# Experts two to four: the first product of two token tiles by seven block products in place of eight

## The reference

```python
def _moe_ref(x, domain_probs, w1, w2):        # N, D, E, F = 1152, 512, 4, 1024
    p = domain_probs / (domain_probs.sum(-1, keepdims=True) + 1e-09)
    out = np.zeros((N, D), dtype=np.float32)
    for e in range(E):
        h = np.maximum(x @ w1[e], 0.0)
        out += p[:, e:e + 1] * (h @ w2[e])
    return out.astype(np.float32)

def _moe2_ref(x, w_in, w_out):                # d_ff = 2048
    h = x @ w_in
    g = h * np.cos(h)
    return (g @ w_out).astype(np.float32)
```

## Time and profile before

| | us |
|---|---|
| median of three runs | 654.84 |
| the profiled execution | 654.78 |
| its span, first to last instruction | 653.0 |
| TensorE busy with matmuls | 642.1 |
| weight loads of TensorE | 576.5 |
| VectorE busy | 259.6 |
| ScalarE busy | 235.7 |
| GpSimd busy | 163.6 |
| granted TensorE clock | 1.000 of full |

### The profile page before, as it was taken

One profiled execution on the slowest core, in us unless ns is written; L12 is line 12 of the kernel. 1 busy time (PEld: TensorE's weight loads), 2 busy tenths in 40 slices (PEclk: granted clock), 3 DMA queues, 4 the chain that ended last, 5 costly groups with the idle time before them and its releaser, 6 DMA issues.

```text
span 653.0 us, 10127 instructions
## 1 busy us (share of the span) xinstructions
PE 642.1 (98%) x3728; PEld 576.5 (88%) x3728; DVE 259.6 (40%) x638; ACT 235.7 (36%) x514; POOL 163.6 (25%) x222
## 2 busy tenths in 40 slices
PE   7899999999999999999999999999999999999998
PEld 5787889999999999999999999998999999999996
DVE  6755321212121212121212122316766576767664
ACT  6676311232111133111133111137554567644552
POOL 6683200154000154000055000068300049500000
PEclk9999999999999999999999999999999999999999
DMA  9865100033000044000034000023200003001011
GB/s 288 258 196 150 68 0 1 6 126 127 1 1 0 1 129 128 0 0 0 0 100 153 6 0 1 1 66 106 86 1 1 1 33 97 2 0 48 0 49 48
DMA packets 21892, 37.21 MB, mean 57 GB/s; under 512 B 2784, under 2 KB 14048, under 8 KB 21856
## 3 DMA queue, kind: packets, MB, share of 16 engines
q1 hardware_dynamic: 20688, 36.71, 17.7%
q10 hardware_dynamic: 1168, 0.02, 0.1%
HBM read 34.36 MB, written 2.36 MB: 56 GB/s over the span
## 4 chain that ended last, share of the span: by engine, by line
PE 96%; DVE 2%; issue 1%; ACT 1%; DMA 1%; POOL 0%; SPq 0%; DVEq 0%
PE bank L865 46%; PE bank L892 45%; PE bank L857 2%; PE bank L821 1%; PE bank L841 1%; DVE arena L613 1%; PE bank L911 1%; DMA arena<-in_k 1%; ACT arena L440 0%; DVE arena L690 0%; DVE arena L628 0%; ACT x_hi L453 0%; POOL arena L387 0%; DVE arena L633 0%; SPq L248 0%
## 5 line engine op out<-in xcount | busy, mean ns | idle before, releaser
L361 POOL TENSOR_TENSOR w_lo<-w_raw,w_hi 128x128 fp32r<-128x128 f32 (+2 forms) x180 | 138.1, 798 | 370.5 <-ACT w_hi L471 368.4
L865 PE MATMUL bank<-x_hi,w_hi 128*128 128x384 f32 (+1 forms) x576 | 196.9, 342 | 0.0
L865 PE MATMUL bank<-x_hi,w_lo 128*128 128x384 f32 (+1 forms) x576 | 194.7, 338 | 0.0
L865 PE MATMUL bank<-x_lo,w_hi 128*128 128x384 f32 (+1 forms) x576 | 193.5, 336 | 0.0
L892 PE MATMUL bank<-w_hi,hp_hi 128*128 128x512 f32 x432 | 170.9, 396 | 0.1
L892 PE MATMUL bank<-w_hi,hp_lo 128*128 128x512 f32 x432 | 170.3, 394 | 0.0
L892 PE MATMUL bank<-w_lo,hp_hi 128*128 128x512 f32 x432 | 168.1, 389 | 0.0
L647 DVE SCALAR_TENSOR_TENSOR hp_lo<-bank,hp_hi 128x384 fp32r<-128x384 f32 x96 | 53.3, 557 | 264.4 <-ACT hp_hi L476 264.4
L476 ACT ACTIVATE hp_hi<-bank 128x384 fp32r<-128x384 f32 x96 | 46.9, 491 | 278.1 <-PE bank L865 275.8
L865 PEld LDWEIGHTS bank<-x_hi,w_hi 128*128 128x128 f32 x576 | 108.3, 188 | 7.1 <-issue 1.0
L865 PEld LDWEIGHTS bank<-x_lo,w_hi 128*128 128x128 f32 x576 | 108.3, 188 | 4.9
(11 more groups left out here) (55 smaller groups left out, 346.2 us busy)
## 6 DMA issues: line engine op xcount, KB each, us to landing
w_raw<-in_weights SPq DMA_DIRECT2D x43, 512.0 KB, 3.6
arena<-in_q SPq DMA_DIRECT2D x12, 192.0 KB, 4.8
result<-arena SPq DMA_DIRECT2D x9, 256.0 KB, 2.1
w_raw<-in_weights SPq DMA_DIRECT2D x8, 256.0 KB, 6.3
arena<-in_k SPq DMA_DIRECT2D x8, 224.0 KB, 5.9
arena<-in_v SPq DMA_DIRECT2D x4, 384.0 KB, 5.1
arena<-in_v SPq DMA_DIRECT2D x4, 320.0 KB, 8.1
arena<-in_k SPq DMA_DIRECT2D x4, 192.0 KB, 3.6
```

Source lines behind the costliest of these rows:

```text
L361: last = nc.gpsimd.tensor_tensor(w_lo[:, f, at:at + part], raw[:, at - begin:at - begin + part], w_hi[:, f, at:at + part], ALU.subtract)
L865: last = nc.tensor.matmul(ps[:, 0:TOK], w[:, f, chunk(c)], x[:, c, token_cols(t)], start=c == 0 and i == 0, stop=c == DC - 1 and i == 2)
```

## The change

For experts 2 to 4 (e = 1 to 3) the first product of tiles 0 and 1 is taken for two chunks of features at once, by Strassen's method in Winograd's form. A is the two chunks' weights (rows: chunk 2g, chunk 2g + 1; columns: the first and second half of the 512 inner elements), B is x (rows: the halves; columns: tile 0, tile 1). Seven products of [256 inner] x [128 features] x [384 tokens], each 2 pieces x 3 matmuls, give the four cells (chunk, tile). The eight products of the kernel before were these 2 x 2 cells of 12 matmuls. The third tile is still done alone, and the first expert and the dense block keep their form.

- **Sums of x (T)**: 10 sums of 128x768 and 4 low parts of that size on POOL, 4 roundings on ACT (`t_high`), once, in the first expert's second and third turns. The fourth overwrites `x_hi` and `x_lo` of tile 1's first half.
- **Sums of weights (S)**: per pair of chunks ("group") 4 sums of 128x256 in place in `w_raw` (`sum_weights`), 2 roundings of 128x512 on ACT (`high_sums`), 4 low parts of 128x256 on POOL (`low_sums`). A slot is loaded again only after its sums are split (`ex_lo_done`). POOL's `low_weights` for the experts is cut from 1024 columns to 256.
- **Combining**: the products alternate between banks 0 and 1. ACT copies the first to `h_raw` (`keep_first`), DVE adds the other six in seven instructions (`add`, L924). ReLU and rounding read `h_raw` (`pair_high`, L630), and so does `pair_low` (L908), now with both operands in SBUF.
- **Second product**: tile 0 sums up in banks 2, 3 and 7, tile 1 in banks 4, 5 and 6, nine matmuls per cell as before. Tile 0's and tile 1's results are taken in the third tile's turn, the third tile's in the next expert's first group, or, after the last expert, in the dense block's start.
- **Third tile**: `pe_alone` runs up in banks 0 and 1 and down two chunks behind. Its last two downs stand in the next expert's first group, or between the dense block's first ups.

The core of the diff:

```diff
-            with pe.Fori(1, E - 1) as e:
-                with pe.Fori(0, NTOK - 1) as t:
-                    pe_turn(e, t, e * NTOK + t)
-                pe_turn(e, NTOK - 1, e * NTOK + NTOK - 1)
-            pe_turn(E - 1, 0, MIX - NTOK)
-            for t in range(1, NTOK):
-                pe_turn(E - 1, t, MIX - NTOK + t, inputs=True)
+            with pe.Fori(1, E - 1) as e:
+                pe_pairs(e)
+                pe_alone(e)
+            pe_pairs(E - 1)
+            pe_alone(E - 1, inputs=True)
+
+            pe.wait_ge(x2_lo_done, OC)
+            for f in range(LAG):
+                pe.wait_ge(w_lo_done, E * FC + f + 1)
+                if f < 2:
+                    pe.wait_ge(hp_lo_done, MIX * FC - 1 + f)
+                up_cells(h_ps[f], f, 0, range(DC)).then_inc(up_done, 1)
+                if f < 2:
+                    down(FC - 2 + f, MIX * FC - 2 + f, None)
             pe_turn(E, 0, MIX, inputs=True)
...
+            def pair_product(g, j, left, right):
+                for c in range(2):
+                    (a_hi, a_lo), (b_hi, b_lo) = left(c), right(c)
+                    for i, (a, b) in enumerate(((a_hi, b_hi), (a_hi, b_lo), (a_lo, b_hi))):
+                        last = nc.tensor.matmul(bank[(g * PRODUCTS + j) % 2][:, 0:TOK], a, b,
+                                                start=c == 0 and i == 0, stop=c == 1 and i == 2)
+                last.then_inc(pair_up, 1)
...
+                    pair_product(g, 0, a11, b11)
+                    pe.wait_ge(ex_lo_done, ex_count(e, g, 0))
...
+                    pair_product(g, 1, s2, t2)
+                    if g == 0:
+                        down(FC - 2, alone(e - 1) * FC + FC - 2, None)
+                    else:
+                        pair_outputs(e, g - 1, 2)
+                    pe.wait_ge(ex_lo_done, ex_count(e, g, 1))
+                    pe.wait_ge(first_kept, kept_count(e, g))
+                    pair_product(g, 2, s1, t1)
+                    pe.wait_ge(pair_taken, product_count(e, g, 0))
+                    pair_product(g, 3, a12, b21)
+                    if g == 0:
+                        down(FC - 1, alone(e - 1) * FC + FC - 1, None)
+                    else:
+                        pair_outputs(e, g - 1, 3)
+                    pe.wait_ge(pair_taken, product_count(e, g, 1))
+                    pair_product(g, 4, s4, b22)
+                    pe.wait_ge(pair_taken, product_count(e, g, 2))
+                    pair_product(g, 5, s3, t3)
+                    pair_outputs(e, g, 0)
+                    pe.wait_ge(w_lo_done, e * FC + (2 * g + 2))
+                    pe.wait_ge(pair_taken, product_count(e, g, 3))
+                    pair_product(g, 6, a22, t4)
+                    pair_outputs(e, g, 1)
...
+            def high_sums(e, g):
+                act.wait_ge(s_summed, e * (GROUPS * 4) + (4 * g + 4))
+                for half in range(2):
+                    nc.scalar.activation(ex_hi[:, g, half * DM:(half + 1) * DM], w_raw[:, (2 * g + half) % STAGE, 0:DM],
+                                         ACT.Copy).then_inc(ex_hi_done, 1)
...
+                for g in range(GROUPS):
+                    keep_first(e, g)
+                    pair_high(e, g, 0)
+                    if g + 1 < GROUPS:
+                        high_sums(e, g + 1)
+                    pair_high(e, g, 1)
+                    pair_high(e, g, 2)
+                    if g < 2:
+                        high_weights(4 + 2 * g, e, alone(e - 1))
+                    pair_high(e, g, 3)
+                    if g < 2:
+                        high_weights(5 + 2 * g, e, alone(e - 1))
...
+            for i in range(LAG):
+                if i < LAG - 1:
+                    times_cosine(i, MIX * FC + i, i > 0)
+                else:
+                    times_cosine(i, MIX * FC + i, True, take_last_of_experts)
```

More of the change, by code:

```diff
@@ L134, in build @@
[L134 to L148, removed]
+        acc = sb("acc", [P, NTOK, DC * TOK])
@@ new lines, in act_alone @@
+            def act_alone(e, sums):
+                for f in range(FC):
+                    alone_high(e, f)
+                    if not sums:
+                        if f >= LAG:
+                            high_weights(f - LAG, e + 1, alone(e))
+                    elif f in (3, 4, 5):
+                        high_weights(f - 3, e + 1, alone(e))
+                    elif f == 6:
+                        high_sums(e + 1, 0)
+                    elif f == 7:
+                        high_weights(3, e + 1, alone(e))
+                    if not sums and f >= 2:
+                        next_input_high(f - 2)
@@ L510, in act_turn @@
                         continue
[L512 to L518 removed]
+                    refill = (f - 1, e + 1, turn) if refills and f > 0 else None
+                    cosine(g, s, True, refill)
                     if inputs and f in TURNS:
@@ L521, in act_turn @@
                 if refills:
[L522 removed]
+                    high_weights(FC - 1, e + 1, turn)
             exponentials(0, 0)
@@ L678, in take_outputs, with dve_alone @@
+            def dve_alone(e, inputs=False):
+                for f in range(FC):
+                    hidden_low(f, alone(e) * FC + f, bank[f % 2])
+                    if f == 0:
+                        take_pair_tile(e, SECOND_TILE)
+                    elif f == 1:
+                        take_pair_tile(e, FIRST_TILE)
+                    if inputs and f >= 2:
+                        next_input_low(f - 2)
             def take_outputs(e, turn, t, last=False):
@@ new lines, in pe_alone @@
+            def pe_alone(e, inputs=False):
+                for f in range(FC):
+                    if f < 2:
+                        pe.wait_ge(pair_taken, product_count(e, GROUPS - 1, 5 + f))
+                    else:
+                        pe.wait_ge(hp_lo_done, alone(e) * FC + (f - 1))
+                    up_cells(bank[f % 2], f, NTOK - 1, range(DC)).then_inc(up_done, 1)
+                    if f < 2:
+                        pair_outputs(e, GROUPS - 1, 2 + f)
+                    else:
+                        down(f - 2, alone(e) * FC + f - 2, tile_taken(e, SECOND_TILE))
+                    if inputs and f >= 2:
+                        turn_input(f - 2)
```

460 lines of the change are left out of this document (349 added, 111 removed).

## The result

| | before | after |
|---|---|---|
| median | 655.16 us (5 runs, 654.76 to 656.16) | 650.68 us (5 runs, 649.98 to 652.42) |
| ratio | 1 | 0.9932, 95% interval 0.9915 to 0.995 |
| profiled execution | 654.78 us, span 653.0 | 650.12 us, span 648.2 |

The changed kernel is faster by 0.7%, or 4.5 us. The prediction was 644.2 us with a range of 642.0 to 647.0, so the sign was right and 5.9 us of the profiled execution's time were not foreseen.

A forecast was written before the change was run, and what follows sets the result against it. TensorE, busy 98% of the span, was taken to bound the kernel, so each removed matmul gives back its whole spacing: 654.78 - 12.64 (matmuls removed) + 2.05 (wait at the dense block's start) = 644.2 us, range 642.0 to 647.0.

The forecast's parts named there:

- What is removed: Groups of experts 2 to 4: 72 first-product matmuls of 384 columns go, at 0.1756 us each, a gain of 12.64 us.
- What stays: Second products: still 9 matmuls for each chunk and tile, a step taken at 2.06 us, with no cost added.
- Rival E: Products of six matmuls are spaced wider: 0.03 us more for each of 504, 15 us, 659 in all; chance 0.02.
- Inside a group: Groups of 15.6 us: bank and cell hand-overs have 1.5 to 2.3 us of slack, so they cost nothing.
- Rival B: Round trips bind in the groups: each of 12 waits some 0.3 us, 647.8 us in all; chance 0.09.
- GpSimd: Some 105 us more GpSimd work; tightest at an expert's first use of the weight sums, slack 1.5 us, cost nothing.
- Rival C: GpSimd is late by up to 3 us at each expert's first product needing its sums: 645 to 647 us; chance 0.08.
- rival D: GpSimd runs lock VectorE's `pair_low` out, 4 us in each of 9 groups: 36 us, 680 in all; chance 0.03.
- The start of the dense block: A down waits 2.27 us for VectorE's take (2.37 with a slower first matmul); net cost 2.05 us.
- U: The end of the third dense chunk's up on TensorE; the down waiting for VectorE's take was to begin 4.38 us later.
- The sum: Whole kernel: 654.78 - 12.64 + 2.05 = 644.2 us, against the profiled execution's own time.

## Why the prediction was wrong, point by point

- **What is removed: right.** 72 matmuls fewer, the first product's spacing unchanged, a run of six in 1.06 us as the earlier trace rows had it.
- **What stays: the step that failed.** "Second products stay at 9 for each chunk and tile" was true of their number, and the sum silently kept their 2.06 us. They took 2.10, as `hp` had moved by 32 bytes against `w` and `x`. The sum lacked a term, for which no row of before gave a price: 4.9 us by the medians with and without the move (650.68 - 645.8). The profiled executions differ by 4.25 us, or by 4.6 from VectorE's `x_lo` row near 84 us to the end; ahead of it the second one ran its first 20 us at a granted clock of 0.91. Rival E spoke of wider spacing, but of the products of six, and at 0.02.
- **Inside a group: right in kind.** TensorE waits nowhere in them. Against 15.61 us a group took 15.78, and 15.66 with `hp` in its old place, so 12 x 0.05 = 0.6 us are left over. Rival B would have shown waits and did not come.
- **GpSimd: right.** 269.0 - 163.6 = 105.4 us more, against 105. The first low sums began at 140.32, 0.7 us a piece, so the first two were ready at 141.7; TensorE took the first of their products at 143.41. Slack 1.7 us, against 1.5. Rival C did not come.
- **`pair_low` and rival D: right for the instruction looked at.** The row below gives 0.59 us on average, and the longest took 1.01, within 0.55 to 1.3. But the block was looked for only in `pair_low`. The copy of shares stood at 85.16 in the trace of before, and the text itself put the first sum at 84.8. A small instruction behind a large one of GpSimd: 1.4 us late, 0.5 us for TensorE. The Trainium skill, page SBUF — State Buffer, section Who interferes with whom, names copies among the instructions that can take the pair of ports which VectorE shares with GpSimd, with the second to come blocked for the whole instruction. By that rule, the trace agrees: 1.56 us, up to the end of the sum.
- **The start of the dense block: right.** Predicted was a down at U + 4.38, and it began at U + 4.37; predicted were 2.27 us of waiting, and it was 2.28 by the starts. The reason held too: moving the take alone gave the time back, 2.5 us against 2.05 predicted as its net cost (2.37 with the 0.32 that the kernel before lost as well). Not seen was that the clock can fall behind the wait, which cost 1.5 us in two other executions.
- **The sum.** 136 second products stand behind the first tile's turn, 48 of them in the 12 groups. 644.2, plus 12 x 0.17 = 2.0 for the groups, 88 x 0.04 = 3.5 for the other second products and 0.5 for the copy, is 650.2, against 650.12 measured. With the placement of before the change gives 645.8 us, inside the range; without the move of `hp` the prediction would have been 1.6 us low. Of these, 0.6 are in the groups and 0.5 are the copy; the last 0.5 has no name.

In the changed kernel, `pair_low` by line, and GpSimd's timeline at the first low sums:

```profile
L908 DVE SCALAR_TENSOR_TENSOR hp_lo<-h_raw,hp_hi 128x384 fp32r<-128x384 f32 x48 | 28.5, 593 | 14.7 <-ACT hp_hi L630 14.7
```

```profile
140.32 2.83 POOL L536 TENSOR_TENSOR ex_lo<-w_raw,ex_hi 128x256 fp32r<-128x256 f32 x4
```

## What to carry to other kernels

When a kernel is bound by TensorE, compare the spacing of the matmuls that were not edited before explaining a result: a tile that grew by 24 bytes shifted an operand and took back more than a third of a gain of 12.6 us. Keep the distances between the operand tiles when tiles are added (put new ones behind them), and try a few shifts of 32 bytes; they cost no instruction. Before moving the steps of a waiting engine, follow the chain back: here cosines on other engines set the time, and only moving the take forward among them helped. Price a wait of a busy TensorE at more than its length if other runs show its clock falling behind one.

## What was not expected of the hardware

- The spacing of fp32r matmuls, with a weight load before each, depends on how far the stationary and the moving operands stand apart in SBUF: 9 matmuls of 512 columns took 2.04 to 2.10 us, 12 of 384 took 2.10 to 2.12, for shifts of 32 to 128 bytes at full clock. In the kernel before and in the changed kernel it came out the same in the experts and in the dense block, and shifts by 256 and 512 bytes left it as it was. The Trainium skill, page TensorE: Matmul & The Clock Gate, section Back-to-back issue gap, gives N / 2.4 + 2.5 ns for a lone matmul and has no term for place. An estimate by it is 1.94 us for nine, which no placement here reached.
- After TensorE had stood idle for 2.16 and 2.17 us its granted clock fell to about 0.5 in two of seven executions, and 1.5 us were lost beyond the wait; in the other five it stayed at 1.00.
- One sum of 128x768 on GpSimd held a VectorE copy of 128x3 from SBUF to SBUF for 1.4 us. The rounding `hp_lo` just ahead of it, which started 0.16 us before the sum and reads a bank and SBUF, kept its 0.55 us.
